# A fused linear-attention and gated-layers kernel: lead-in loads of two tokens per row, turned in 64 by 64 tiles, with ScalarE storing y

## The reference

```python
y[:, :, t] = np.einsum('bhd,bhde->bhe', rt, state)
Sa = np.einsum('bhde,bhe->bhd', state, at)
state_decay = state * wt[:, :, None, :] - np.einsum('bhd,bhe->bhde', Sa, bt)
state = state_decay + np.einsum('bhd,bhe->bhde', vt, kt)
```

## Time and profile before

| | us |
|---|---|
| three runs | 895.15, 901.50, 901.98 |
| median | 901.5 |
| profiled execution: device time | 899.85 |
| profiled execution: span from first to last instruction | 898.1 |
| attention, by the last y product (L626) | 0 to about 454 |
| lead-in, up to the first product of chunk 0 (L692) | 0 to 84.70 |

### The profile page before, as it was taken

The page is one execution under the profiler, slowest core; times in us unless marked ns, Lnnn a source line. Parts: engine busy times, 40 slices in busy tenths (PEclk is TensorE's granted clock), DMA queues, the critical chain, the costliest instruction groups (busy, mean ns, idle before and its releaser), DMA issues.

```text
span 898.1 us, 29931 instructions
## 1 busy us (share of the span) xinstructions
PE 798.4 (89%) x13477; PEld 736.9 (82%) x13477; DVE 509.5 (57%) x705; ACT 390.0 (43%) x521; POOL 306.3 (34%) x475
## 2 busy tenths in 40 slices
PE   3878778889989897888899998999989999899997
PEld 3767677778878786776788998999989999899997
DVE  3969556557675553232358468534775347753484
ACT  1212333433434344343456176622757137561374
POOL 4188988078186188820012200212002020030200
PEclk9869898988999988799999999999999999999999
DMA  9999567288466444734260010100101000010001
GB/s 115 122 115 134 93 121 112 67 138 108 100 111 117 80 102 99 166 72 72 63 188 1 1 36 18 45 1 1 36 19 45 1 4 33 25 38 1 1 1 44
DMA packets 236219, 59.37 MB, mean 66 GB/s; under 512 B 226336, under 2 KB 231356, under 8 KB 236092
## 3 DMA queue, kind: packets, MB, share of 16 engines
q1 hardware_dynamic: 173948, 47.94, 26.8%
q10 hardware_dynamic: 62144, 9.51, 8.1%
HBM read 43.01 MB, written 14.42 MB: 64 GB/s over the span
## 4 chain that ended last, share of the span: by engine, by line
PE 45%; DVE 12%; ACT 9%; issue 5%; DMA 1%; SPq 0%; ACTq 0%; DVEq 0%
PE p L1026 26%; PE p L671 6%; DVE stage L1313 6%; ACT big L1218 3%; DVE big L1232 3%; PE p L1118 2%; PE p L769 2%; ACT stage L1213 2%; PE p L795 1%; PE p L736 1%; PE p L779 1%; PE p L814 1%; PE p L692 1%; PE p L829 1%; PE p L756 1%
## 5 line engine op out<-in xcount | busy, mean ns | idle before, releaser
L449 POOL TENSOR_TENSOR prod<-t_pair 128x30 f32<-128x30 f32 (+9 forms) x180 | 108.1, 601 | 81.9 <-DMA t_pair<-m_scratch 67.9
L1328 POOL TENSOR_TENSOR big<-stage,big 128x1024 fp32r<-128x1024 f32 x12 | 28.8, 2400 | 286.3 <-DVE stage L1268 286.3
L1026 PE MATMUL p<-xs,w 128*128 128x384 f32 x560 | 110.5, 336 | 5.8 <-ACT tmp L1206 5.8
L452 POOL TENSOR_TENSOR t_pair<-t_pair,prod 128x30 f32<-128x30 f32 (+9 forms) x180 | 107.5, 597 | 14.1
L1026 PEld LDWEIGHTS p<-xs,w 128*128 128x128 f32 x560 | 98.4, 188 | 7.3 <-ACT tmp L1206 6.9
L1026 PE MATMUL p<-wo,big 128*128 128x320 f32 x576 | 95.5, 325 | 9.2 <-DVE big L1232 9.0
L1026 PEld LDWEIGHTS p<-wo,big 128*128 128x128 f32 x576 | 91.5, 200 | 12.4 <-DVE big L1232 11.1
L1026 PE MATMUL p<-wsg_hi,big 128*128 128x384 f32 x384 | 98.6, 335 | 2.2 <-ACT stage L1180 1.9
L1026 PEld LDWEIGHTS p<-wsg_hi,big 128*128 128x128 f32 x384 | 69.6, 188 | 3.2 <-ACT stage L1180 2.6
L1313 DVE SCALAR_TENSOR_TENSOR stage<-tmp,cols,stage 128x768 f32<-128x768 f32 x48 | 48.4, 1016 | 12.9 <-ACT stage L1210 12.1
L829 PE MATMUL p<-a_t,kb_t 40*128 40x64 f32 x768 | 52.2, 289 | 3.6 <-issue 3.6
(11 more groups left out here) (149 smaller groups left out, 1659.4 us busy)
## 6 DMA issues: line engine op xcount, KB each, us to landing
raw_r<-in_r_dram SPq DMA_DIRECT2D x48, 80.0 KB, 3.3
vp<-in_v_dram ACTq DMA_DIRECT2D x96, 40.0 KB, 2.4
x_scratch<-y_t SPq DMA_DIRECT2D x48, 80.0 KB
out_dram<-stage SPq DMA_DIRECT2D x11, 320.0 KB, 2.3
m_scratch<-n_t SPq DMA_DIRECT2D x48, 64.0 KB
t_pair<-m_scratch SPq DMA_DIRECT2D x6, 512.0 KB, 5.1
t_scratch<-t_pair SPq DMA_DIRECT2D x6, 512.0 KB, 4.1
t_sb<-t_scratch SPq DMA_DIRECT2D x24, 128.0 KB
```

The costliest lines, as they stand in the source:

```text
L449: pool.tensor_tensor(p_v, tp[:, 0:s, s:s + 1].to_broadcast([PAIRS, s, n]), tp[:, s:s + 1, s + 1:C].to_broadcast([PAIRS, s, n]), ALU.mult). ...
L452: pool.tensor_tensor(tp[:, 0:s, s + 1:C], tp[:, 0:s, s + 1:C], p_v, ALU.add).then_inc(elim, 1)
L1026: last = pe.matmul(out_of(p, half), l, r, start=step == 0 and first, stop=step == steps - 1 and not part)
L1328: pool.tensor_tensor(dst, src, hi.bitcast(F32), ALU.subtract).then_inc(sem_, 1)
```

## The change

Four things are changed.

1. In the first five pairs (`HEAD`, units 0 to 9) a partition of `raw` holds two consecutive tokens of one batch, so that a DMA writes 32 partitions and pieces of 80 words (320 bytes). TensorE turns them in 64 by 64 tiles: per head one tile for the even and one for the odd tokens of each pair of batches, 16 operations for four heads where there were 4. Those in the lower half of the partitions are transposes, those in the upper half plain products with the identity, and the two kinds alternate. The results are written to PSUM with a column stride of two words, so the layout behind is as it was. Units from 10 on are turned as before.
2. In steps -1 to 7 both scans of w take their second operand, a tile of ones and zeros, from PSUM, and the forward scan writes to PSUM.
3. The lead-in is reordered: SP issues b and a of the next pair ahead of the stores of `n_t` for units 0 to 7, and ACT issues the second halves of k and a after its first two copies of w, k of pair 1 a step later, and a of pair 1 behind the first `kb_n`.
4. ScalarE issues the stores of y, at the end of its own step, instead of SP.

```diff
-        def load_half(eng, src, n, half, s):
-            hs = slice(4 * half, 4 * half + 4)
+        one_psum = p0[:, 0]
+        def scan_place(u):
+            if u <= R_LAG:
+                return p0[:, 1].rearrange("p (n t) -> p n t", t=C), one_psum
+            return e_scan[:], w_one
+        def load_rows(eng, src, n, pair, s, hs=slice(0, H)):
+            toks = slice(pair * 2 * C, (pair + 1) * 2 * C)
             for bt in range(B):
                 bi, be = bt // 2, bt % 2
-                eng.dma_start(raw[n][0][be * HP:(be + 1) * HP, hs, bi, 0:D],
-                              src[bt, hs, 0:2 * C, :].rearrange("h p d -> p h d")).then_inc(s, 16)
+                if pair < HEAD:
+                    eng.dma_start(as_pairs(raw[n][pair % 2])[bt * C:(bt + 1) * C, hs, 0:2 * D],
+                                  src[bt, hs, toks, :].rearrange("h (p q) d -> p h (q d)", q=2)).then_inc(s, 16)
+                else:
+                    eng.dma_start(raw[n][pair % 2][be * HP:(be + 1) * HP, hs, bi, 0:D], src[bt, hs, toks, :].rearrange("h p d -> p h d")).then_inc(s, 16)
...
+            def next_pair(u):
+                if u % 2 == 1 and u // 2 + 2 < NU // 2:
+                    if u // 2 + 2 >= HEAD:
+                        sp.wait_ge(k_full, u + 1)
+                        load(k, "k", u // 2 + 2, k_in)
+                    sp.wait_ge(b_full, u + 1)
+                    load(b, "b", u // 2 + 2, b_in)
+                    sp.wait_ge(a_full, u + 1)
+                    load(a, "a", u // 2 + 2, a_in)
             for s in range(NC + LAG + 2):
                 u = unit(s - 1)
                 if u is not None:
+                    if u < R_LAG:
+                        next_pair(u)
...
-                if u is not None:
-                    if u % 2 == 1 and u // 2 + 2 < NU // 2:
...
+                if u is not None and u >= R_LAG:
+                    next_pair(u)
...
+                cy = chunk(s - LAG - 1)
+                if cy is not None and cy % 2 == 1:
+                    act.wait_ge(y_done, cy + 1)
+                    for be, bi in SIDES:
+                        rows = x_t[2 * bi + be].rearrange("(h e) s -> e h s", e=D)[:, :, (cy - 1) * C:(cy + 1) * C]
+                        act.dma_start(rows, y_t[bi * HP:bi * HP + D, :, be, :]).then_inc(gm.x0_out if cy == NC - 1 and bi + be == 0 else y_out, 16)
...
-            def four(buf, half):
-                return [buf[:, 4 * half + j].rearrange("p i d -> p (i d)") for j in range(4)]
+            def turned(bank, buf, un):
+                if un // 2 >= HEAD:
+                    return transposes(bank, [buf[:, 4 * (un % 2) + j].rearrange("p i d -> p (i d)") for j in range(4)])
+                for j in range(4):
+                    for odd in range(2):
+                        for bi in range(2):
+                            rows = slice(bi * HP, (bi + 1) * HP)
+                            out_cols = free(bank[rows], j * P + odd, [[HP, 2], [2, C]])
+                            tile = as_pairs(buf)[rows, 4 * (un % 2) + j, odd * D:odd * D + HP]
+                            if bi:
+                                last = pe.matmul(out_cols, tile, ident[rows, rows], start=True, stop=True)
+                            else:
+                                last = pe.transpose(out_cols, tile, ident[rows, rows])
+                return last
```

More of the change, by code:

```diff
@@ L272, in load @@
             def load(src, n, pair, s):
-                for bt in range(B):
-                    bi, be = bt // 2, bt % 2
-                    sp.dma_start(raw[n][pair % 2][be * HP:(be + 1) * HP, :, bi, 0:D], rows_of(src, bt, pair)).then_inc(s[pair % 2], 16)
+                load_rows(sp, src, n, pair, s[pair % 2])
             def load_r(v_):
@@ L464, in load_side @@
             def load_side(src, n, pair, s):
[L465 to L468, removed]
+                load_rows(act, src, n, pair, s[pair % 2])
             load_first(act, k, "k", k_in)
             load_first(act, a, "a", a_in)
-            load_second(act, k, "k", k_in)
-            load_second(act, a, "a", a_in)
             act.wait_ge(mask_step, 5)
@@ L506, in _ @@
                 if s == -1:
+                    load_second(act, k, "k", k_in)
+                    load_second(act, a, "a", a_in)
+                if s == 0:
                     load_side(k, "k", 1, k_in)
-                if s == 0:
-                    load_side(a, "a", 1, a_in)
                 if 5 <= s < 5 + RV:
@@ L712, in _ @@
                         pe.wait_ge(kbn_out, u)
-                    transposes(p3[:, 0], four(raw["w"][pair % 2], un % 2)).then_inc(w_full, 1)
+                    turned(p3[:, 0], raw["w"][pair % 2], un).then_inc(w_full, 1)
                 if u is not None:
@@ L720, in _ @@
                     wait_raw(pe, "k", k_in, u)
-                    transposes(p2[:, 1], four(raw["k"][pair % 2], u % 2)).then_inc(k_full, 1)
+                    turned(p2[:, 1], raw["k"][pair % 2], u).then_inc(k_full, 1)
                     if un is None:
@@ L724, in _ @@
                     wait_raw(pe, "b", b_in, u)
-                    transposes(p3[:, 1], four(raw["b"][pair % 2], u % 2)).then_inc(b_full, 1)
+                    turned(p3[:, 1], raw["b"][pair % 2], u).then_inc(b_full, 1)
                     wait_raw(pe, "a", a_in, u)
-                    transposes(p2[:, 0], four(raw["a"][pair % 2], u % 2)).then_inc(a_full, 1)
+                    turned(p2[:, 0], raw["a"][pair % 2], u).then_inc(a_full, 1)
                 if c is not None:
```

30 lines of the change are left out of this document (20 added, 10 removed).

## The result

The changed kernel takes 1066.57 us (median of 4 runs, 1066.15 to 1067.27), the kernel before 899.61 on the same chip (4 runs): 1.1858 times as long, with a 95% interval of 1.1801 to 1.1916. It is slower, as forecast. But the forecast was 960 with a range that ended at 1025, and the time lies 42 us beyond that. The profiled execution took 1066.93 us, its span is 1065.2.

A forecast was written before the change was run, and what follows sets the result against it. VectorE sets the lead-in step now; TensorE would become the bound. 899.85 + 50.7 (chunk 0 later) + 6.8 (step 9) - 7.7 (waits) + 9.3 (clock) + 1 (y stores) = 960 us, range 905 to 1025.

The forecast's parts named there:

- The bound: Lead-in: TensorE becomes the bound at 13.8 us a step, with VectorE's 6.6 us beside it.
- The mechanism of the turning: Turning in 64 by 64 tiles: TensorE empties at each change between transpose and product, and each instruction is such a change.
- The price of a pair: One transpose and product in the turning: 0.34 us, bounds 0.25 to 0.51; 2.7 us a tensor against 0.44.
- The clock: TensorE in the nine lead-in steps: 0.93 of full clock over 124.2 us, counted as +9.3 us.
- Rival D: The clock stays at 1.2 GHz through the lead-in, so 124.2 and 13.6 us are added: 1082 us; chance 0.06.
- Rival B: No handover cost between the tiles, both kinds side by side, 1.0 us a tensor: faster, 889 us; chance 0.13.
- rival C: Handovers paid only once per pair, pair 0.2 us, tensor 1.7: 915 us, span 903 to 935; chance 0.11.
- Step 9 and the waits: Three more tensors turned in step 9, +6.8 us; waits of 4.41 for r and 3.29 for `t_sb` go, -7.7 us.
- y on ScalarE: ScalarE issues the y stores; five fall into steps without units, at most 5 x 0.9 us; taken as +1 us.
- Scans in PSUM: Lead-in scans may change by some tenths either way, covered by VectorE's 7 us to spare a step: 0 us.
- a clock near 0.5: Sign in the new profile: a lead-in clock near 0.5 would show the forecast wrong.

The follow-up runs named there:

- Grouping: The changed kernel, but in each turned tensor the eight transposes come first and then the eight products: 976.41 us, 1.0846 of the kernel before.
- the run of transposes alone: The changed kernel with 16 upper-corner transposes in a row per tensor; only w's lower corner turned, by products; twelve whole transposes first: 955.94 us, 1.0609.

## Why the prediction was wrong, step by step

- **The bound.** Right. TensorE becomes it, VectorE waits for it in every step, and TensorE has no wait for b or a. One reading on the way was loose: a DMA share of 0.97 was called not full without a reason. (Between 40 and 50 us of the same trace it reads 1.42.)
- **The mechanism of the turning.** Right in kind: a change between transpose and product is paid each time. Grouping takes most of the changes away and 90 us with them.
- **The price of a pair.** Mis-sized. It was summed to 0.34 us at full clock and is 0.43, inside the bounds of 0.25 and 0.51. With 3.44 us a tensor the step is 4 x 3.44 + 2.92 = 16.7 us. With w begun at 5.8, the first w and its copies done at about 10.6 and 0.6 for r, chunk 0 would be at 161.5: +76.8 instead of +50.7. The term was 26 us short, with the clock still taken as full. The Trainium skill's rule that a change of tiling mode drains TensorE (TensorEngine Tiling (Array Packing), Key Properties) stood beside this term without a price; the pair's rows are in line with it.
- **The clock: the step that failed.** "I take 0.93, a bit above the 0.89 of now", for 9.3 us. TensorE ran at 1.2 GHz up to chunk 0. A pair is 0.64 and the rest of the step 5.36, and chunk 0 comes at 246.0 and not at 161.5: 84.5 us. The working took full clock as given and let it fall only where TensorE had waited. But the clock was low from the first instruction on, as the earlier trace rows had it with 1.09 us for four transposes, and nothing in the lead-in raised it. Nor would full clock have lasted: with w alone in pairs it fell in eight steps without a wait, and the run of transposes alone shows a stream that stays low. What in the corner's work does this is open, as said there.
- **The sum with these in it.** 960 + 26 for the pair, 84.5 - 9.3 = 75 for the clock, and 5.8 in place of the 0.1 that was forecast from chunk 0 on (6.8 - 7.7 + 1), give 1067.
- **Rival D** had the right mechanism and 1082 us, with a chance of 0.06. It doubled the whole price of a pair; a pair gets 1.5 times as long (0.43 to 0.64). Its two errors, 0.34 for a pair and the doubling, nearly cancel. The reason against it, that TensorE doesn't wait here, was no reason: the clock fell without a wait where only w was in pairs.
- **Rival B** needed both kinds to run side by side. The kernel with products alone does what B says, at 0.94 us a tensor, and takes 885 to 889 us where B gave 889. (In rival C eight pairs of 0.2 us are 1.6 and not 1.7, which makes its 915 some 4 us too high.) The mistake in the kernel is the kind of the upper corner's operation, not the idea of the tiles.
- **Step 9 and the waits.** +6.8 was worked out at 2.72 us a tensor; at 5.12 it is 3 x 4.68 = +14.0. The waits for r and `t_sb` fall from 10.1 to 2.5 us from chunk 0 on, so -7.6, as the -7.7 said. Together +6.4, measured +5.8. The closeness is in part luck. Step 9 grew from 16.9 us (84.70 to 101.63) to 30.2 (246.02 to 276.20), by 13.3 where 14.0 - 4.4 = 9.6 follows, since TensorE stayed at 1.2 GHz behind the three tensors as well: `kb_t` in that step takes 1.94 us. The steps after it were shorter by about as much again.
- **y on ScalarE.** +1 was taken. The comparison, 888.88 against 889.99, neither shows nor refutes an effect of that size.
- **Scans in PSUM.** 0 fits here, where GpSimd waits 74.4 and 63.0 us for its input anyway; no run of the changed kernel has its scans in SBUF. The reason given looked at VectorE alone. Where TensorE isn't the bound the scans are worth about 1% of the time, through GpSimd.

What decided the size was a price that the trace before could bound and did, and a condition of the clock that it couldn't show, because no stretch of it had such work in it. The forecast said what would refute it, a clock near 0.5; the chance of that should have been large, since the trace gave no row of such small transposes at either level of the clock, and its first rows were at the lower one.

## What to carry to other kernels

Small pieces in opposite corners of TensorE are worth it if all of them are products: 32 passes take 0.94 us at 2.4 GHz. The 24 that alternate with transposes take 3.44 at that clock, and 5.12 at the 1.2 GHz that they ran at. When work of a kind that no row shows goes onto the engine that will be the bound, give the lower clock a real chance and work out that case in full. Read the clock off the length of a known instruction before believing a column of 1.00 at the start of a trace.

## What the hardware showed that was not expected

- TensorE went from 2.4 to 1.2 GHz while it was busy without a gap, in pairs of a transpose in one 64 by 64 corner and a product in the opposite one. One tensor of such pairs was enough for it in each of eight steps, and in the products in both corners behind them it came back (0.43 to 0.59 us a pair, then 0.053 and 0.029 us a pass).
- A stream made up mostly of transposes in one corner stayed at 1.2 GHz for some 130 us without a wait (16 of them in 1.71 us, against 1.08 at first). With whole transposes TensorE rose to 2.4 GHz (20 in 4.2 us, then 46 in 5).
- The record of the clock reads 1.00 until its first change, at either level: for the whole lead-in of the changed kernel, where eight transposes took 1.97 us and not 1.06.
- A scan on VectorE with both inputs in SBUF holds up GpSimd until it is over: 31.3 us for 60 instructions against 21.1 with the ones in PSUM.
- Four loads in pieces of 80 words on 32 partitions take 1.8 to 1.9 us on SP's queue; in pieces of 40 words on 64 partitions, with the same bytes, they took 2.6 to 3.0. The first two of the sync queue before and after the change:

```profile
0.80 3.02 SPq L252 DMA_DIRECT2D stage<-in_w_dram  x4
3.86 2.63 SPq L252 DMA_DIRECT2D stage<-in_b_dram  x4
```

```profile
0.80 1.82 SPq L265 DMA_DIRECT2D stage<-in_w_dram  x4
2.66 1.86 SPq L265 DMA_DIRECT2D stage<-in_b_dram  x4
```
